# Attention scores on TensorE: even and odd heads in the lower and the upper 64 rows of the array, each with a PSUM bank of its own

## The chip, the cores and the metric

The kernel runs on one core of a Trainium2 chip. The metric is the device time of one execution in microseconds (us), as the median of several runs. The profile is one further execution, recorded by the hardware profiler; its span is the time from the first to the last recorded instruction of the core. TensorE stands in it as two engines: PE is the matmul itself and PEld the load of the stationary operand (LDWEIGHTS), which overlaps the matmul before it. The others are VectorE (DVE), ScalarE (ACT), GpSimd (POOL) and SyncE (SP), which issues the DMAs.

## The reference

Pooled attention over 4 batches, 8 heads, 576 tokens and a head size of 64, followed by two feed-forward layers over the 2304 tokens. All numbers are float32.

```
k_p = k.reshape(B, H, Sp, pool, D).mean(axis=3)          # pool = 8, Sp = 72
v_p = v.reshape(B, H, Sp, pool, D).mean(axis=3)
scores = scale * np.matmul(q, k_p.transpose(0, 1, 3, 2))
scores = scores - np.max(scores, axis=-1, keepdims=True)
attn = np.exp(scores)
attn = attn / (np.sum(attn, axis=-1, keepdims=True) + 1e-09)
x = np.matmul(attn, v_p)                                  # then to (2304 tokens, 512)
xn = x / sqrt(mean(x * x) + 1e-06) * rms_g
x = (silu(xn @ w_gate) * (xn @ w_val)) @ w_out            # 512 -> 1536 -> 512
h = x @ w_in;  y = silu(h) @ w_out                        # 512 -> 2048 -> 512
```

## The kernel before

The first tenth of the time is the attention; the rest are the two feed-forward layers, whose matmuls (line 2010 and the lines behind it) keep TensorE busy to the end. The change touches the attention alone.

The 2304 tokens are cut into 18 tiles of 128. A batch has 576 tokens, four and a half tiles, so tiles 4 and 13 hold tokens of two batches: `parts(n)` gives two parts of 64 tokens for them and one part of 128 for each other tile. The list `order`, written out at the start of the kernel, sets what each engine does; all engines walk through the same list. In step s it has: the scores of tile s, the transposes of tile s-1's probabilities (`prT`), the transposes of the queries of tile s+1 (`q`), the transposes of the normalized output of an earlier tile (`x`), for three tiles the transposes of a new batch's keys (`keys`), and the product with the values of tile s-1 (`pv`). So on TensorE one round is: scores (line 1909), `prT` (line 1921), `q` (line 1896), `x` (line 1953), `pv` (line 1940), and then the scores of the next tile.

The other engines work between these. ScalarE copies the transposed queries from PSUM to `qT` (line 1411) and the pooled keys to `kT` (line 1394), makes the exponentials in place in `pr` (line 1086) and copies their transpose to `prT` (line 1420). VectorE takes the maximum of the scores for each head (line 1487, into `mx`), subtracts it (line 1492, into `pr`), and divides the product with the values by the sums (lines 1507 to 1514). Semaphores order all this; `s_sc` counts the score tiles made, `s_shift` the tiles subtracted.

The scores of one part are four matmuls, one for each pair of heads c. The stationary operand is `qT[:, c, tokens]`: partitions 0 to 63 hold the 64 elements of the even head, 64 to 127 those of the odd head. The moving operand is a block of `kT` of 128 partitions and 144 columns, block-diagonal: the even head's 72 keys stand in the lower 64 partitions and columns 0 to 71, the odd head's in the upper 64 partitions and columns 72 to 143, and the other two quarters are zero. VectorE clears both `kT` buffers once at the start (line 1809) and the copies fill only the two quarters. The scores of heads 0 to 3 lie in PSUM bank 2 and those of heads 4 to 7 in bank 3. One float32 matmul of the code stands in the trace as two pairs of LDWEIGHTS and MATMUL, so the scores of a tile are 8 pairs, those of tiles 4 and 13 are 16.

In the trace, a TensorE instruction carries its rows and columns of the array: 128\*128 uses all of it, 128\*64 only 64 columns, as the matmuls for the 64-token parts of tiles 4 and 13 do, in the scores and in the product with the values.

Of the kernel before, what the change touches and what calls it, by code (L numbers as in the profile page):

```python
# [13 lines left out]
P = 128  # L14
# [6 lines left out]
def ffn_kernel(nc, q, k, v, w_gate, w_val, w_out, rms_g, w2_in, w2_out, out):  # L21
    B, H, S, D = q.shape
    DM = H * D
    KC = DM // P
    T = B * S
    SP = S // POOL
# [21 lines left out]
    def parts(n):  # L48
        at, found = n * P, []
        while at < (n + 1) * P:  # L50
            b = at // S
            end = min((b + 1) * S, (n + 1) * P)
            found.append((b, at - n * P, end - at))
            at = end
        return found

    order = [("q", 0)]
    for s in range(NT + 2):
# [228 lines left out]
    with ctx:  # L287
# [6 lines left out]
        def sem(name):  # L294
            return ctx.enter_context(nc.semaphore(name))
# [77 lines left out]
            vb.append(at(spot, f"vb{i}", [P, RC, HS, E]))  # L373
            spot += 4 * RC * HS * E
        for i in range(2):
            kT.append(at(spot, f"kT{i}", [P, R]))
            spot += 4 * R
        assert spot <= ring_at[2] + SLOT
        spot = c_at + RAW
        ident = at(spot, "ident", [P, P])  # L380
# [97 lines left out]
        o_ps = ps[:, 6:8, 0:HB * E].rearrange("p b (h e) -> p b h e", e=E)  # L478

        s_const, s_mask, s_ident = sem("const_made"), sem("mask_made"), sem("ident_made")  # L480
        s_pad0, s_pad, s_clear = sem("k0_pad_cleared"), sem("pad_cleared"), sem("kT_pr_cleared")
        s_q = [sem(f"q_loaded{i}") for i in range(2)]
        s_k = [sem(f"k_loaded{i}") for i in range(2)]
        s_v = [sem(f"v_loaded{i}") for i in range(2)]
# [40 lines left out]
        def _(sp):  # L525
# [31 lines left out]
            def load_raw(i):  # L557
                kind, x = made[i]
                if raw_before[i] is not None:
                    sp.wait_ge(s_wlo, raw_before[i] + 1)  # L560
                elif raw_of(i) == 2:
                    sp.wait_ge(s_sc, NT)
                elif made[i] == ("r", U2 + 1):

                    sp.wait_ge(s_flo, PART * 4)
                elif kind == "c" and CHOME[x] == 0:
                    sp.wait_ge(s_out, 16)
                elif kind == "c":
                    sp.wait_ge(s_down, down0[ND])
                    sp.wait_ge(s_ost[0], o_store[o_maker[GROUPS[1] + GROUPS[2] - 1]])  # L570
                    sp.wait_ge(s_ost[1], o_store[o_maker[GROUPS[1] + GROUPS[2] - 2]])
                elif raw_of(i) >= 7:
                    sp.wait_ge(s_prod, NF * (last_unit[0] + 1))
                elif raw_of(i) > 3:
                    sp.wait_ge(s_ksum, 3)
                    sp.wait_ge(s_vsum, 3)
                if made[i] in (("r", U2 + 2), ("o", N2)):
                    sp.wait_ge(s_wh, 2 * (NF - 1))
                if made[i] == ("c", 6):
                    sp.wait_ge(s_wh, 4 * NF)  # L580
                if kind == "b":

                    sp.dma_start(raw[raw_of(i)][:, :].rearrange("p (k n) -> p k n", k=2),
                                 w_out.rearrange("(k j p) n -> p j k n", p=P, k=2)[:, x, :, :])\
                      .then_inc(s_raw[raw_of(i)], 16)
                elif kind == "c":
                    sp.dma_start(raw[raw_of(i)][:, :].rearrange("p (k n) -> p k n", k=2),
                                 w2_out.rearrange("(k j p) n -> p j k n", p=P, k=2)[:, x, :, :])\
                      .then_inc(s_raw[raw_of(i)], 16)
                elif kind == "r":  # L590
                    ph, letter, g, _ = units[x]
                    sp.dma_start(raw[raw_of(i)][:, :].rearrange("p (c n) -> p c n", c=KC),
                                 up_v[letter][:, :, g * FF:(g + 1) * FF]).then_inc(s_raw[raw_of(i)], 16)
                else:
                    g = downs[x][1]
                    sp.dma_start(raw[raw_of(i)][:, :].rearrange("p (c n) -> p c n", c=2),
                                 down_v[ffn_of[x]][:, 2 * g:2 * g + 2, :]).then_inc(s_raw[raw_of(i)], 16)
# [485 lines left out]
        def _(act):  # L1083
# [302 lines left out]
            def keys(b):  # L1386

                act.wait_ge(s_kTm, b + 1)
                act.wait_ge(s_clear, 3)
                if b >= 2:  # L1390
                    act.wait_ge(s_sc, first_tile[b - 1] + 1)
                for e in range(2 if b else 1):
                    half = slice(e * D, (e + 1) * D)
                    last = act.activation(
                        kT[b % 2][half, :].rearrange("p (c e j) -> p c e j", e=2, j=SP)[:, :, e, :],
                        flat[half, 0:R].rearrange("p (c e j) -> p c e j", e=2, j=SP)[:, :, e, :], ACT.Copy)
                last.then_inc(s_kTc, 1)

# [7 lines left out]
            for what, n in order:  # L1406
                if what == "q":
                    act.wait_ge(s_qTm, n + 1)
                    if n >= 1:
                        act.wait_ge(s_sc, n)  # L1410
                    act.activation(qT[:, :, :], q_ps, ACT.Copy).then_inc(s_qTc, 1)
                    if n in first_tile:
                        keys(first_tile.index(n))
                    if n >= 1:
                        exp(n - 1)
                elif what == "prT":
                    act.wait_ge(s_pTm, n + 1)
                    if n >= 1:
                        act.wait_ge(s_o, n)
                    act.activation(prT[:, :, :], prT_ps, ACT.Copy).then_inc(s_pTc, 1)  # L1420
                    if n == NT - 2:
                        exp(NT - 1)
                    if n == NT - 1:
                        keep_first(0)
                elif what == "pv":
                    if n >= 2:
                        norm(n - 2)
                    if n >= 1:
                        squares(n - 1)
                    if n in (8, 9, 13):  # L1430
                        weight_high(0, ((8, 9, 13).index(n),))
                    if n in (15, 16, 17):
                        weight_high(made_at["r", 1], (n - 15,))
                elif what == "x" and 7 <= n < 7 + NF:
                    token_high(0, XORDER[n - 7])
                elif what == "unit":
                    act_unit(n)
# [25 lines left out]
        def _(dve):  # L1463
# [17 lines left out]

            def shift(n):
                scores = sc_ps.rearrange("p b (h j) -> p b h j", j=SP)
                dve.wait_ge(s_sc, n + 1)
                if n >= 1:
                    dve.wait_ge(s_shift, n)
                dve.tensor_reduce(mx[:, :].rearrange("p (b h) -> p b h", b=2), scores, AX.X, ALU.max)\
                   .then_inc(s_max, 1)
                dve.wait_ge(s_max, n + 1)
                if n >= 2:  # L1490
                    dve.wait_ge(s_pTm, n - 1)
                dve.tensor_tensor(pr[:, n % 2, 0:R].rearrange("p (b h j) -> p b h j", b=2, j=SP), scores,
                                  mx[:, :].rearrange("p (b h) -> p b h", b=2).unsqueeze(3)
                                  .broadcast_to([P, 2, HB, SP]), ALU.subtract).then_inc(s_shift, 1)

# [309 lines left out]
                    ending_low(ENDINGS.index(ph), 0, ((0, 1), (2, 3))[g - EPART - 1])  # L1805

            dve.memset(KV[0][0][LAST:P, RC - 1, :], 0.0).then_inc(s_pad0, 1)
            for i in range(2):
                dve.memset(kT[i][:, :], 0.0).then_inc(s_clear, 1)
            dve.memset(pr[:, :, R:RC * P], 0.0).then_inc(s_clear, 1)  # L1810
            for i in range(2):
                dve.wait_ge(s_kpart[i], 16)
# [2 lines left out]
            sum_rows(0, *KPARTS[2]).then_inc(s_kpartsum, 1)  # L1815

            dve.wait_ge(s_kTm, 1)
            dve.wait_ge(s_clear, 3)
            dve.tensor_copy(kT[0][D:2 * D, :].rearrange("p (c e j) -> p c e j", e=2, j=SP)[:, :, 1, :],
                            flat[D:2 * D, 0:R].rearrange("p (c e j) -> p c e j", e=2, j=SP)[:, :, 1, :])\  # L1820
               .then_inc(s_khalf, 1)
            for what, n in order:
# [53 lines left out]
        def _(pe):  # L1876
# [23 lines left out]
            def scores(n):  # L1900
                pe.wait_ge(s_qTc, n + 1)
                pe.wait_ge(s_kTc, parts(n)[-1][0] + 1)
                if n == 0:
                    pe.wait_ge(s_khalf, 1)
                else:
                    pe.wait_ge(s_shift, n)
                for b, r0, m in parts(n):
                    for c in range(KC):
                        last = pe.matmul(sc_ps[r0:r0 + m, c // 2, (c % 2) * 2 * SP:(c % 2 + 1) * 2 * SP],  # L1909
                                         qT[:, c, r0:r0 + m], kT[b % 2][:, c * 2 * SP:(c + 1) * 2 * SP],  # L1910
                                         start=True, stop=True)
                last.then_inc(s_sc, 1)

            def transpose_p(n):
                pe.wait_ge(s_exp, n + 1)
                pe.wait_ge(s_clear, 3)
                if n >= 1:
                    pe.wait_ge(s_pTc, n)
                pe.wait_ge(s_kTc, sum(1 for b in range(B) if first_tile[b] <= n + 1))
# [285 lines left out]
```

## Time and profile before

| | |
|---|---|
| time, median of 3 runs | 861.84 us (861.83 to 861.92) |
| the profiled execution's own time | 861.54 us |
| its span | 859.8 us |
| instructions in it | 13900 |
| PE busy | 850.9 us (99%) |
| PEld busy | 830.6 us (97%) |
| DVE busy | 551.4 us (64%) |
| ACT busy | 359.9 us (42%) |
| POOL busy | 422.4 us (49%) |
| data moved by DMA | 235.78 MB |

Busy time is the time in which at least one instruction of the engine is under way, from its start to its end; for PE that includes the time in which a result still runs through the array, so that overlapping matmuls are not counted twice.

### The profile page before, as it was taken

What the parts mean: (1) busy time and instruction counts of PE and PEld (TensorE: products, weight loads), DVE (VectorE), ACT (ScalarE), POOL (GpSimd) and SP (SyncE); (2) the same over time, 40 slices, a digit from 0 to 9 for tenths busy, and PEclk for the clock granted to TensorE, in tenths of its full rate; (3) what the DMA queues carried; (4) which work ended last, traced back from release to release, by engine and by line L of the source; (5) the groups of instructions that cost most, each with busy time, mean ns of one, the idle gap of its engine ahead of it and who ended that gap; (6) DMA issues with size and microseconds to landing.
All of it is one profiled execution on the core that took longest, in us unless ns stands there. A gap on an engine that the chain in (4) does not pass through costs nothing.

```text
span 859.8 us, 13900 instructions
## 1 busy us (share of the span) xinstructions
PE 850.9 (99%) x5292; PEld 830.6 (97%) x5292; DVE 551.4 (64%) x835; ACT 359.9 (42%) x640; POOL 422.4 (49%) x415
## 2 busy tenths in 40 slices
PE   7999999999999999999999999999999999999998
PEld 6999999999999999999899899999999999999998
DVE  6789757876545579965554345569634698335873
ACT  3689745443221335555553221324333444134521
POOL 6898999883427480577773044380161700004400
PEclk9999999999999999999999999999999999999999
DMA  9971578778869987565779489997789747687763
GB/s 266 277 203 39 221 267 325 269 297 315 335 213 405 409 327 264 201 262 221 282 289 370 160 295 363 356 401 266 265 288 359 255 188 285 248 335 244 257 232 114
DMA packets 95201, 235.78 MB, mean 274 GB/s; under 512 B 23072, under 2 KB 69920, under 8 KB 83616
## 3 DMA queue, kind: packets, MB, share of 16 engines
q1 hardware_dynamic: 95136, 234.90, 75.4%
q8 instruction: 42, 0.69, 0.3%
q14 instruction: 23, 0.19, 0.1%
HBM read 164.10 MB, written 70.78 MB: 273 GB/s over the span
## 4 chain that ended last, share of the span: by engine, by line
PE 97%; DVE 1%; DMA 1%; issue 0%; ACT 0%; SPq 0%; DVEq 0%
PE ps L2010 17%; PE ps L2012 17%; PE ps L2011 17%; PE ps L2148 5%; PE ps L2147 5%; PE ps L2146 5%; PE ps L1940 4%; PE ps L2106 3%; PE ps L2107 3%; PE ps L2108 3%; PE ps L2077 3%; PE ps L2078 3%; PE ps L2076 3%; PE ps L1909 2%; PE ps L2052 2%; PE ps L2053 2%
## 5 line engine op out<-in xcount | busy, mean ns | idle before, releaser
L2010 PE MATMUL ps<-xh,wr 128*128 128x384 f32 x840 | 283.2, 337 | 0.3
L2012 PE MATMUL ps<-xh,wr 128*128 128x384 f32 x840 | 281.4, 335 | 0.0
L2011 PE MATMUL ps<-xl,wr 128*128 128x384 f32 x840 | 281.2, 335 | 0.0
L2010 PEld LDWEIGHTS ps<-xh,wr 128*128 128x128 f32 x840 | 157.7, 188 | 4.4 <-DVE qt L1579 1.5
L2011 PEld LDWEIGHTS ps<-xl,wr 128*128 128x128 f32 x840 | 157.9, 188 | 0.3
L2012 PEld LDWEIGHTS ps<-xh,wr 128*128 128x128 f32 x840 | 157.7, 188 | 0.0
L2148 PE MATMUL ps<-ew,efl 128*128 128x256 f32 x336 | 95.2, 283 | 0.0
L2147 PE MATMUL ps<-ew,efh 128*128 128x256 f32 x336 | 95.2, 283 | 0.0
L2146 PE MATMUL ps<-ew,efh 128*128 128x256 f32 x336 | 95.2, 283 | 0.0
L1598 DVE TENSOR_TENSOR qt<-ps,qt 128x384 f32<-128x384 f32 x84 | 46.3, 556 | 49.8 <-PE ps L2012 49.7
L959 POOL TENSOR_TENSOR eh<-eh 128x768 f32<-128x768 f32 x8 | 17.2, 2168 | 122.5 <-DVE efl L1675 122.5
L2148 PEld LDWEIGHTS ps<-ew,efl 128*128 128x128 f32 x336 | 64.6, 192 | 0.0
L2146 PEld LDWEIGHTS ps<-ew,efh 128*128 128x128 f32 x336 | 64.6, 192 | 0.0
L2147 PEld LDWEIGHTS ps<-ew,efh 128*128 128x128 f32 x336 | 64.6, 192 | 0.0
L1188 ACT ACTIVATE qt<-ps 128x384 f32<-128x384 f32 x42 | 20.6, 492 | 101.4 <-PE ps L2012 100.9
L1675 DVE TENSOR_TENSOR efl<-eh,efh 128x768 fp32r<-128x768 f32 x56 | 59.8, 1123 | 5.1 <-ACT efh L1288 5.1
L939 POOL TENSOR_TENSOR ebt<-raw_z 128x256 f32<-128x256 f32 x8 | 5.9, 737 | 112.7 <-PE ps L2108 39.9
L1288 ACT ACTIVATE efh<-eh 128x768 fp32r<-128x768 f32 x56 | 43.0, 834 | 41.3 <-PE ps L2148 41.3
L2106 PE MATMUL ps<-fh,fw 128*128 128x384 f32 x168 | 56.2, 334 | 0.0
L2107 PE MATMUL ps<-fl,fw 128*128 128x384 f32 x168 | 56.2, 334 | 0.0
L2108 PE MATMUL ps<-fh,fw 128*128 128x384 f32 x168 | 56.2, 334 | 0.0
L1587 DVE TENSOR_TENSOR qt<-ps,qt 128x384 f32<-128x384 f32 x42 | 23.4, 558 | 51.0 <-PE ps L2012 51.0
(198 smaller groups left out, 1769.0 us busy)
## 6 DMA issues: line engine op xcount, KB each, us to landing
wr<-ring_home SPq DMA_DIRECT2D x40, 1792.0 KB, 9.7
ring_home<-wr SPq DMA_DIRECT2D x20, 1792.0 KB, 8.1
ew<-ending_home SPq DMA_DIRECT2D x8, 2048.0 KB, 8.5
out_home<-wo SPq DMA_DIRECT2D x14, 1024.0 KB, 9.4
fw<-fold_home SPq DMA_DIRECT2D x8, 1536.0 KB, 7.8
ew<-out_home SPq DMA_DIRECT2D x24, 512.0 KB, 7.5
fw<-out_home SPq DMA_DIRECT2D x18, 512.0 KB, 6.6
ending_home<-eb SPq DMA_DIRECT2D x16, 512.0 KB, 10.7
```

The source lines that it names most:

```text
L1288: act.activation(efh[e][i % 2][:, 2 * j:2 * j + 2, :], ending_part(f, j), ACT.Copy).then_inc(s_ehi, 1)
L1598: dve.tensor_tensor(done if units[u][1] == "V" else qt[:, c, :], done, tiles(u)[:, c, :], ALU.add)\
L1675: dve.tensor_tensor(efl[e][i % 2][:, 2 * j:2 * j + 2, :], ending_part(f, j), efh[e][i % 2][:, 2 * j:2 * j + 2, :], ALU.subtract).then_inc( ...
L2010: pe.matmul(out_ps, w_hi, x_hi, start=first and c == 0, stop=False, skip_group_check=True)
L2011: pe.matmul(out_ps, w_hi, x_lo, start=False, stop=False, skip_group_check=True)
L2012: ins = pe.matmul(out_ps, w_lo, x_hi, start=False, stop=c == 1, skip_group_check=True)
L2106: pe.matmul(out_ps, w_hi, h_hi, start=first and c == 0, stop=False, skip_group_check=True)
L2107: pe.matmul(out_ps, w_hi, h_lo, start=False, stop=False, skip_group_check=True)
L2108: ins = pe.matmul(out_ps, w_lo, h_hi, start=False, stop=c == 2 * PART - 1, skip_group_check=True)
L2146: pe.matmul(out_ps, h_hi, w_hi, start=first and c == 0, stop=False, skip_group_check=True)
L2147: pe.matmul(out_ps, h_hi, w_lo, start=False, stop=False, skip_group_check=True)
L2148: ins = pe.matmul(out_ps, h_lo, w_hi, start=False, stop=c == 2 * EPART - 1, skip_group_check=True)
```

## The change

Each of the four score matmuls of a part becomes two, one for the even head (e = 0) and one for the odd head (e = 1). A matmul takes only the 64 partitions of its head, of `qT` and of `kT`, and makes 72 columns instead of 144. The even head's operands lie in partitions 0 to 63 and so in the one half of the array's rows, the odd head's in the other half. Even heads' scores go to PSUM bank 2 and odd heads' to bank 3.

`kT` keeps only the filled quarters: it is 4 × 72 columns wide in each half of the partitions instead of 8 × 72, its copies write 288 columns in a row, and the two clears of line 1809 go. The subtraction reads the scores bank by bank as before but writes `pr` in the order of the heads, with jumps of 72. `s_sc` now rises by two for each part (once for each bank), and `scored(n)` gives the count that stands for n tiles.

```diff
+    def scored(n):
+        return sum(2 * len(parts(i)) for i in range(n))
...
-            kT.append(at(spot, f"kT{i}", [P, R]))
-            spot += 4 * R
+            kT.append(at(spot, f"kT{i}", [P, HB * SP]))
+            spot += 4 * HB * SP
...
                 act.wait_ge(s_kTm, b + 1)
-                act.wait_ge(s_clear, 3)
...
                     last = act.activation(
-                        kT[b % 2][half, :].rearrange("p (c e j) -> p c e j", e=2, j=SP)[:, :, e, :],
+                        kT[b % 2][half, :].rearrange("p (c j) -> p c j", j=SP),
                         flat[half, 0:R].rearrange("p (c e j) -> p c e j", e=2, j=SP)[:, :, e, :], ACT.Copy)
...
-                dve.wait_ge(s_sc, n + 1)
+                dve.wait_ge(s_sc, scored(n + 1))
...
-                dve.tensor_tensor(pr[:, n % 2, 0:R].rearrange("p (b h j) -> p b h j", b=2, j=SP), scores,
+                dve.tensor_tensor(pr[:, n % 2, 0:R].rearrange("p (h b j) -> p b h j", b=2, j=SP), scores,
...
-            for i in range(2):
-                dve.memset(kT[i][:, :], 0.0).then_inc(s_clear, 1)
...
                 for b, r0, m in parts(n):
                     for c in range(KC):
-                        last = pe.matmul(sc_ps[r0:r0 + m, c // 2, (c % 2) * 2 * SP:(c % 2 + 1) * 2 * SP],
-                                         qT[:, c, r0:r0 + m], kT[b % 2][:, c * 2 * SP:(c + 1) * 2 * SP],
-                                         start=True, stop=True)
-                last.then_inc(s_sc, 1)
+                        for e in range(2):
+                            ins = pe.matmul(sc_ps[r0:r0 + m, e, c * SP:(c + 1) * SP], qT[e * D:(e + 1) * D, c, r0:r0 + m],
+                                            kT[b % 2][e * D:(e + 1) * D, c * SP:(c + 1) * SP], start=True, stop=True)
+                            if c == KC - 1:
+                                ins.then_inc(s_sc, 1)
```

Nothing changes its place in the order of an engine. On TensorE this is the place from the product with the values of tile 3 over the scores of tile 5 to the transposes behind them, in the kernel before (the form is output columns of a matmul of the code: partitions of the output x moving columns):

```order
L1940 MATMUL ps<-vb,prT 128x65
L1909 MATMUL ps<-kT,qT 128x144 [waits shifted,kT_copied,qT_copied]
L1909 MATMUL ps<-kT,qT 128x144 x3
L1921 MATMUL ps<-ident,pr 128x128 [waits prT_copied,kT_copied,kT_pr_cleared,exp_made]
```

The same place in the changed kernel, in which line 1909 has become 1911, 1921 has become 1923 and 1940 has become 1942:

```order
L1942 MATMUL ps<-vb,prT 128x65
L1911 MATMUL ps<-kT,qT 128x72 [waits shifted,kT_copied,qT_copied]
L1911 MATMUL ps<-kT,qT 128x72 x7
L1923 MATMUL ps<-ident,pr 128x128 [waits prT_copied,kT_copied,pr_cleared,exp_made]
```

And the scores of tile 4 in the changed kernel, the first of the two tiles that are cut into two parts (before, these were 8 matmuls `64x144`):

```order
L1911 MATMUL ps<-kT,qT 64x72 [waits shifted,kT_copied,qT_copied]
L1911 MATMUL ps<-kT,qT 64x72 x15
```

Four matmuls of 144 columns have become eight of 72, behind the same waits and between the same neighbours; for the two cut tiles, eight have become sixteen.

## Rows read from the trace of the kernel before

**Rows 1.** The page: busy time of the engines, granted clock in 40 slices, chain by engine

```profile
PE 850.9 (99%) x5292; PEld 830.6 (97%) x5292; DVE 551.4 (64%) x835; ACT 359.9 (42%) x640; POOL 422.4 (49%) x415
...
PEclk9999999999999999999999999999999999999999
...
PE 97%; DVE 1%; DMA 1%; issue 0%; ACT 0%; SPq 0%; DVEq 0%
```

**Rows 2.** The chain in order of time, one round: start us, us, what

```profile
56.13 1.69 PE ps L1940 x12
57.82 1.04 PE ps L1909 x8
```

**Rows 3.** The chain, around the matmuls that use 64 of the array's columns

```profile
25.09 1.50 PE ps L1940 x12
26.59 1.67 PE ps L1909 x16
28.27 0.70 PE ps L1921 x5
...
36.42 1.18 PE ps L1909 x8
37.60 0.55 PE ps L1921 x5
...
67.10 1.67 PE ps L1909 x16
...
76.93 1.18 PE ps L1909 x8
```

**Rows 4.** The timeline, single instructions: start us, us, engine, line, operation

```profile
57.49 0.19 PEld L1940 LDWEIGHTS ps<-vb,prT 128*128 128x128 f32 x1
57.60 0.19 PEld L1909 LDWEIGHTS ps<-kT,qT 128*128 128x128 f32 x1
...
26.32 0.27 PE L1940 MATMUL ps<-vb,prT 128*128 128x65 f32 x1
26.52 0.13 PEld L1909 LDWEIGHTS ps<-kT,qT 128*64 128x64 f32 x1
...
36.35 0.19 PEld L1909 LDWEIGHTS ps<-kT,qT 128*128 128x128 f32 x1
```

**Rows 5.** All instructions of line 1909: ns min/median/max, starts, forms

```profile
L1909 PE MATMUL ps<-kT,qT x160: 285/286/390, 10.3 to 86.1; 128*128 128x144 f32 x128, 128*64 128x144 f32 x32
```

**Rows 6.** The timeline of PEld: eight loads of a plain tile, eight of a cut one

```profile
53.45 1.04 PEld L1909 LDWEIGHTS ps<-kT,qT 128*128 128x128 f32 x8
...
26.94 0.56 PEld L1909 LDWEIGHTS ps<-kT,qT 128*64 128x64 f32 x8
```

**Rows 7.** The chain at the start of the kernel

```profile
10.27 1.23 PE ps L1909 x8
...
12.32 0.77 DVE pr L1492
...
15.74 0.30 issue
16.05 1.74 PE ps L1940 x12
```

**Rows 8.** The timeline of VectorE at the start of the kernel

```profile
1.63 1.15 DVE L1809 MEMSET kT<- 128x576 f32 x2 [0.18 <-issue]
...
3.44 1.05 DVE L1465 TENSOR_REDUCE kvp<-kv 128x64 f32<-128x512 f32 x1 [0.52 <-DMA kv<-in_k]
...
13.13 1.97 DVE L1465 TENSOR_REDUCE kvp<-kv 128x128 f32<-128x1024 f32 x1
```

**Rows 9.** VectorE and ScalarE in a round, then busy time of 50 to 80 us (PE, PEld, DVE, ACT, POOL)

```profile
55.68 0.76 DVE L1492 TENSOR_TENSOR pr<-ps,mx 128x576 f32<-128x576 f32 x1
...
56.47 0.69 ACT L1086 ACTIVATE pr<-pr 128x576 f32<-128x576 f32 x1
...
50.00:80.00 30.00, 29.56 (x245) 27.89 (x244) 29.31 (x46) 25.91 (x51) 27.10 (x32) 1.00 0.49 134
```

More of the change, by code:

```diff
@@ L480, in ffn_kernel @@
         s_const, s_mask, s_ident = sem("const_made"), sem("mask_made"), sem("ident_made")
-        s_pad0, s_pad, s_clear = sem("k0_pad_cleared"), sem("pad_cleared"), sem("kT_pr_cleared")
+        s_pad0, s_pad, s_clear = sem("k0_pad_cleared"), sem("pad_cleared"), sem("pr_cleared")
         s_q = [sem(f"q_loaded{i}") for i in range(2)]
@@ L561, in load_raw @@
                 elif raw_of(i) == 2:
-                    sp.wait_ge(s_sc, NT)
+                    sp.wait_ge(s_sc, scored(NT))
                 elif made[i] == ("r", U2 + 1):
@@ L1388, in keys @@
                 act.wait_ge(s_kTm, b + 1)
-                act.wait_ge(s_clear, 3)
                 if b >= 2:
-                    act.wait_ge(s_sc, first_tile[b - 1] + 1)
+                    act.wait_ge(s_sc, scored(first_tile[b - 1] + 1))
                 for e in range(2 if b else 1):
@@ L1409, in _ @@
                     if n >= 1:
-                        act.wait_ge(s_sc, n)
+                        act.wait_ge(s_sc, scored(n))
                     act.activation(qT[:, :, :], q_ps, ACT.Copy).then_inc(s_qTc, 1)
@@ L1817, in _ @@
             dve.wait_ge(s_kTm, 1)
-            dve.wait_ge(s_clear, 3)
-            dve.tensor_copy(kT[0][D:2 * D, :].rearrange("p (c e j) -> p c e j", e=2, j=SP)[:, :, 1, :],
+            dve.tensor_copy(kT[0][D:2 * D, :].rearrange("p (c j) -> p c j", j=SP),
                             flat[D:2 * D, 0:R].rearrange("p (c e j) -> p c e j", e=2, j=SP)[:, :, 1, :])\
@@ L1908, in scores @@
                     for c in range(KC):
-                        last = pe.matmul(sc_ps[r0:r0 + m, c // 2, (c % 2) * 2 * SP:(c % 2 + 1) * 2 * SP],
-                                         qT[:, c, r0:r0 + m], kT[b % 2][:, c * 2 * SP:(c + 1) * 2 * SP],
-                                         start=True, stop=True)
-                last.then_inc(s_sc, 1)
+                        for e in range(2):
[3 more added lines that the diff above has]
+                                ins.then_inc(s_sc, 1)
             def transpose_p(n):
                 pe.wait_ge(s_exp, n + 1)
-                pe.wait_ge(s_clear, 3)
+                pe.wait_ge(s_clear, 1)
                 if n >= 1:
```

## The prediction

> **What bounds the kernel now.** I read the page first: PE is busy for 850.9 of 859.8 us, the chain of work that ended last lies on PE for 97%, and the granted clock is full in every slice [rows 1]. So TensorE sets the end, and a nanosecond that it gains or loses in a stretch without waits is one of the whole. Next I read the chain in order of time through the attention. In a plain round the pieces of PE follow one another without a gap, and the scores are one of them: 1.04 us for 8 pairs of load and matmul [rows 2]. There are 18 such stages between 10 and 87 us. Then I looked for what the trace shows of the array in another shape, because the change puts every score matmul into a new one (64 rows). Rows for that exist: the cut tiles 4 and 13 use 64 of 128 columns, and the chain and the single instructions there tell what it costs to enter and leave a shape, and whether two parts of the array work at the same time [rows 3, 4, 6]. Last, the first two tiles, where PE waits for others [rows 7, 8], and the other engines [rows 9].
>
> **Price of a pair before.** Eight loads of the scores take 1.04 us from the first start to the last end; less the 0.19 of the last, seven steps of 0.12 [rows 4, 6]. A record of a matmul has 286 ns [rows 5], since it includes the way through the array; the step is what counts. The matmuls have 144 columns, so a column costs 0.122/144 = 0.85 ns and the eight take 0.98; the remaining 0.06 of the 1.04 is the end of the first load, which nothing covers [rows 2]. The load of 128 columns has a price of its own: two follow each other after 57.60 - 57.49 = 0.11 us, where the matmuls between them have only 65 columns [rows 4]. The whole stage of line 1940 agrees: its columns (four times 195, 130 and 65) would take 1560 × 0.85 ns = 1.33 us, the chain has 1.50 where it doesn't wait [rows 3], so four short matmuls take 0.10 each instead of 0.055. A matmul of 72 columns costs 0.061 and is thus bound by its load, whose 128 columns (tokens) are what they were.
>
> **Price of a pair after.** A tile has 16 pairs, in two streams of 8, one for each half of the rows. No row shows a matmul on 64 rows. Bounds: if only the columns counted and the halves worked side by side, 8 × 0.061 = 0.49 us; if all 16 loads stood in one line, 15 × 0.11 + 0.06 = 1.71. The nearest rows are those of tile 4, whose two parts use different halves of the columns: eight loads take 0.56 us there [rows 6], (0.56 - 0.13)/7 = 0.06 a step [rows 4, 6] for matmuls of 144 columns that cost 0.12 each in a single stream, so the two halves do work side by side. I take the same for halves of the rows, with each stream bound by its loads: 7 × 0.11 + 0.06 = 0.83 instead of 0.98, **-0.15 us** for each stage.
>
> **Price of the change of shape.** The trace shows it in three kinds. Going from the full array to 64 columns, the first load of the scores starts 0.20 us after the last matmul before it (26.32 to 26.52), while in a plain round it starts 0.11 after the load before it, under running matmuls [rows 4]: the array is emptied first, and the load is then uncovered. Going from 64 columns to the full array with a load of 128 columns, the score stage takes 1.18 instead of 1.04, twice [rows 2, 3]: **+0.14**. Going from 64 columns back to the transposes of line 1921, their stage takes 0.70 instead of 0.55 [rows 3]: **+0.15**. After the change every score stage stands between stages on the full array (line 1940 before, line 1921 behind) and pays both. The Trainium skill says so too ("TensorEngine Tiling (Array Packing)", Key Properties): changing the tiling mode, not only the tile, drains TensorE. By that rule, the trace agrees for columns; for rows no run here shows it. Without it the sum below would be the rival with -3.8 us.
>
> **The sum.** Twelve plain stages (tiles 2, 3, 5, 7 to 12, 14, 16, 17): -0.15 + 0.14 + 0.15 = +0.14 each, **+1.7**. Tiles 6 and 15, at 36.42 and 76.93, enter from 64 columns already, since the product of the cut tile stands before them [rows 3]: -0.15 + 0.15 = **0**. Tiles 4 and 13 pay both changes already, and their loads have 64 columns, about 0.06 us, as their matmuls: 1.67 is 0.15 to enter and 1.52 for 16 pairs, against 1.96 in one line, so the second part began 0.54 us after the first, 4.4 of its 8 pairs [rows 3]. After, each part runs as two streams of 8 × 0.061 = 0.49, and with the same lead of 4.4 pairs (0.27) the stage takes 0.76 instead of 1.52: -0.76 each (bounds: no overlap of the parts -0.54, full overlap -1.03), **-1.5**. Tile 0: PE is idle before it, so entering is free, and leaving falls into the wait for VectorE; the 0.15 goes on through its subtraction [rows 7]: **-0.15**, or nothing if the value sum at 13.13 waits for its load [rows 8]. Tile 1 gains 0.15 and loses it on leaving, and behind it are 0.30 of waiting for VectorE anyway [rows 7]: 0. Sum: +1.7 - 1.5 - 0.15 = +0.05 us. The profiled execution took 861.54 us, so 861.6; it lies 0.3 under the median of the runs, so in their terms **861.9 us**.
>
> **What costs nothing.** The two clears of `kT` took 1.15 us, but VectorE then waits 0.52 for the keys' DMA, which ends when it ends [rows 8]. The copies to `kT` have as many elements. The subtraction writes with jumps of 72; it took 0.76 [rows 9], the maximum, which reads in runs of 72, takes about the same. It ends at 56.44, its tile's exponentials at 57.16, and PE asks for them with the scores at 57.60 and with line 1921 after them: 1.1 us and, one score stage later, about 1.4 us of cover. If it took over 1 us longer, PE would wait in every round. VectorE is busy for 29.31 of 30 us between 50 and 80 [rows 9], so PE could gain little more there than that cover; in the forecast PE gains nothing there before tile 13.
>
> **The rivals.**
> (a) The halves' loads stand in one line: one port feeds the stationary operand. For it: no row shows two row halves at once. Against: the loads of two column halves overlap [rows 6]. Body 1.71 instead of 0.98, +0.73: twelve stages × (0.73 + 0.29) = +12.2, tiles 6 and 15 +1.8, the cut tiles 32 × 0.061 = 1.95 instead of 1.52, +0.9, the first two some +1.3: +16.2, **878.1 us**, slower. It decides from a body of 0.95 us on: 14 stages × 0.12 make 1.7 us, what a measurement can tell.
> (b) Loads overlap but the moving columns don't: 16 × 0.061 = 0.98, no gain against the two changes of shape. 12 × 0.29 + 2 × 0.15 + 0.9 = +4.7, **866.6 us**, slower.
> (c) Going to 64 rows and back empties nothing. Then 14 × -0.15 - 1.5 - 0.15 = -3.75, **858.1 us**. Against it is every change of shape that the trace has.
> (d) A load of 64 rows takes half, and columns bind: body 0.49. 12 × (0.29 - 0.49) + 2 × (0.15 - 0.49) - 1.5 - 0.5 = -5.1, **856.8 us**. For it: 64 columns make a load shorter (0.13 against 0.19 [rows 4]); but those are columns, and here they stay 128. The Trainium skill's table ("TensorEngine Tiling (Array Packing)", Theoretical Speedup) promises up to 2× where a small dimension is at most 64, which would be this case; its page on TensorE ("TensorE: Matmul & The Clock Gate", LDWEIGHTS) says that a load's time goes by columns, not rows, which speaks for my 0.83.
>
> **How the numbers follow.** A measurement of this kernel tells about 0.2% (1.7 us) from no change. Forecast 0.47, with its own range 860.5 to 863.5 (body ±0.06 in 14 stages, cut tiles ±0.25 each); (a) 0.17; (b) 0.10; (c) 0.15; (d) 0.07; 0.04 for what I don't see. The range 856.5 to 868.0 leaves out (a) and a little. Faster is (c), (d) and 0.03 of the forecast: 0.25. Slower is (a), (b), 0.04 of the forecast and half of the rest: 0.33. Same: 0.42.
>
> **What would show it.** In the chain after, line 1911 takes about 1.03 us in a plain round (0.20 to enter, 0.83 body) and line 1923 0.70; 1.91 would be (a), 0.89 with 0.55 behind it (c). Loads of line 1911 come in twos, 0.11 from two to two. The cut tiles' stage takes about 0.9. The stages after 100 us keep their length. I am wrong if row halves don't behave as column halves do, which no row can tell me.

## The result: 2.1 us longer

The changed kernel takes 863.95 us (median of 21 executions, 861.87 to 865.13), the kernel before 861.85 in as many (860.95 to 863.21). The ratio is 1.0018, with a 95% interval of 1.0012 to 1.0024. That is a real loss of 2.1 us, at the edge of the 0.2% that the prediction called no change, and forty times the +0.05 of its sum. The profiled execution took 864.21 us (span 862.5), so it stands 0.3 above its median; the one of before, 861.54, stood 0.3 under its own. One execution of one experiment below (`e2_before_fill`) took 926.14 us with a mean granted clock of 0.852; it is left out.

The page after, the lines that answer to [rows 1]:

```profile
PE 854.0 (99%) x5452; PEld 832.4 (97%) x5452; DVE 550.3 (64%) x833; ACT 359.8 (42%) x640; POOL 421.2 (49%) x415
...
PEclk8999999999999999999999999999999999999999
...
PE 95%; DVE 3%; issue 1%; DMA 1%; ACT 0%; SPq 0%; DVEq 0%
```

Three things differ. There are 160 more matmuls, as written. The first digit of the granted clock is 8 where it was 9. And VectorE holds 3% of the chain, where it had 1%. The prediction had neither the second nor the third.

The chain after, in order of time: the start, the first cut tile (4), one plain round, and the end of the attention (start us, us, what):

```profile
10.10 1.14 PE ps L1911 x16
...
12.05 0.77 DVE pr L1495
12.82 0.14 issue
12.96 1.97 PE ps L1911 x16
14.93 1.26 PE ps L1923 x5
...
17.04 3.08 PE ps L1942 x12
20.12 1.05 PE ps L1911 x16
...
29.25 0.96 PE ps L1911 x27
30.21 0.69 PE ps L1923 x5
...
36.09 2.44 PE ps L1942 x22
38.53 1.05 PE ps L1911 x16
39.58 0.69 PE ps L1923 x5
...
56.28 1.04 PE ps L1911 x16
57.32 0.70 PE ps L1923 x5
...
86.47 0.68 DVE xacc L1503
87.15 1.99 DVE xl L1559
...
95.46 1.58 PE ps L1942 x12
```

Lines have moved: 1911, 1923 and 1942 are the 1909, 1921 and 1940 of before. The plain round is as forecast: scores 1.04 as in [rows 2], line 1923 0.70 instead of 0.55 [rows 3]. The cut tile's scores take 0.96 where they took 1.67 [rows 3]. But between 12.96 and 20.12 every stage takes nearly twice its usual time: 1.97 against 1.05, 1.26 against 0.70, 3.08 against about 1.7. The busy time by stretch says why. Columns: stretch, its length, busy us and instructions of PE, PEld, DVE, ACT, POOL, granted clock, DMA share, GB/s. First after, then before:

```profile
9.00:13.00 4.00, 2.20 (x26) 1.63 (x23) 1.98 (x3) 1.59 (x4) 3.15 (x5) 1.00 1.20 255
13.00:19.60 6.60, 6.60 (x35) 6.13 (x36) 4.11 (x4) 2.47 (x4) 2.82 (x5) 0.50 1.16 279
```

```profile
13.00:19.60 6.60, 5.75 (x46) 5.54 (x46) 5.94 (x9) 2.76 (x5) 3.59 (x6) 1.00 1.14 305
```

The granted clock is 0.50 for 6.6 us, the lower of its two levels (1.2 GHz), and TensorE gets through 35 matmuls in it instead of 46, though those of the scores are now half as wide. Before it fell, TensorE had stood still: the scores of tile 0 and the transposes of line 1896 were done at 11.8, and the scores of tile 1 waited for VectorE until 12.96 (the chain's 0.77 of `pr`). But the kernel before has that wait too, and a slightly longer one. The timelines of PE, before and after, with the idle time in brackets, and the busy time of 9 to 13 us before, to set beside the first row above:

```profile
13.23 1.22 PE L1909 MATMUL ps<-kT,qT 128*128 128x144 f32 x8 [1.30 <-DVE pr L1492]
...
12.96 1.97 PE L1911 MATMUL ps<-kT,qT 64*128 64x72 f32 x16 [1.16 <-DVE pr L1495]
```

```profile
9.00:13.00 4.00, 2.28 (x16) 1.64 (x14) 1.90 (x3) 1.50 (x3) 3.29 (x5) 1.00 1.21 276
```

TensorE waited for 1.30 us before and for 1.16 after, and in the four microseconds it was busy for 2.28 and 2.20. So neither the wait nor the busy time tells the two kernels apart; what differs up to there is above all how the scores of tile 0 are made.

The other place is 87.15. Subtracting `xl` on VectorE took 1.99 us of the chain. The same operation on the same tile, with GpSimd's subtraction beside it, in the timelines of before (first fence) and after:

```profile
84.49 0.95 DVE L1556 TENSOR_TENSOR xl<-xt,xh 128x768 fp32r<-128x768 f32 x1
84.51 2.06 POOL L900 TENSOR_TENSOR wr<-wt,wr 128x512 fp32r<-128x512 f32 x1
```

```profile
87.05 1.27 POOL L904 TENSOR_TENSOR wr<-wt,wr 128x512 fp32r<-128x512 f32 x1
87.07 2.07 DVE L1559 TENSOR_TENSOR xl<-xt,xh 128x768 fp32r<-128x768 f32 x1
```

Before, VectorE began 0.02 us ahead of GpSimd, took 0.95, and GpSimd took 2.06. After, GpSimd began 0.02 ahead, took 1.27, and VectorE took 2.07. They don't share the time; the later one waits. Its time is nearly the rest of the first one's and its own in a row: 1.25 + 0.95 = 2.20 us for the 2.07 of VectorE, and 0.93 + 1.27 = 2.20 for the 2.06 of GpSimd. The Trainium skill has this rule ("SBUF — State Buffer", SBUF: two separate sides): VectorE and GpSimd share one pair of ports, "an exclusive lock, not a bandwidth split", and the one that starts first holds it for its whole instruction. By that rule, both traces agree on who waits, though a lead of 0.02 us decides it; the waiting one ends 0.13 to 0.14 us earlier than a full wait would make it.

**Where 2.67 us between the profiled executions lie.** I read the start of each tile's scores in both timelines. The first scores start 0.17 earlier after (10.10 against 10.27; over all traces here they start between 9.87 and 10.60, whatever the kernel). From tile 0 to tile 2, where the clock is low, 9.95 us instead of 7.35: +2.60. (Two traces of this kind of kernel with the full clock, `e1_fill` and `e12_after_tiny` below, take +0.26 and +0.22 there, so about 2.4 of it are the clock's.) From tile 2 to tile 17, 67.94 instead of 67.58: +0.36. From tile 17 to the last product with the values (before it started at 92.00, after at 95.46), 7.47 instead of 6.80: +0.67, behind the late `xl`. Together 3.46. The rest of the kernel gives 0.79 back, where TensorE waits for others anyway: the distance between the traces is 3.55 us at 127 us, 3.43 at 248, 3.13 at 515 and 2.73 at 776. It shrinks at three places of the kernel before (at 179, 482 and 564 us), by about 0.3 us at each.

### The profile page after: what moved, and what is told of

It is laid out like the page before. It is cut to its first block, busy times and chain, and to the rows that moved or that the text cites. A ratio compares the mean times of both kernels' runs of the same rounds, so it can differ in the third digit from the quotient of the medians.

```text
span 862.5 us, 14215 instructions
## 1 busy us (share of the span) xinstructions
PE 854.0 (99%) x5452; PEld 832.4 (97%) x5452; DVE 550.3 (64%) x833; ACT 359.8 (42%) x640; POOL 421.2 (49%) x415
## 4 chain that ended last, share of the span: by engine, by line
PE 95%; DVE 3%; issue 1%; DMA 1%; ACT 0%; SPq 0%; DVEq 0%
PE ps L2012 17%; PE ps L2014 17%; PE ps L2013 17%; PE ps L2150 5%; PE ps L2149 5%; PE ps L2148 5%; PE ps L2110 3%; PE ps L2109 3%; PE ps L2108 3%; PE ps L1942 3%; PE ps L2079 3%; PE ps L2080 3%; PE ps L2078 3%; PE ps L2055 2%; PE ps L2054 2%; PE ps L2053 2%
```

## Experiments

Each is the changed kernel or the one before with the edit shown. The median of before that stands beside each was taken on the same chip at the same time.

### The cut tiles alone, and the plain tiles alone

`e3_cut_only` scores only tiles 4 and 13 on half rows; the others keep the block-diagonal `kT` and the full array. `e4_plain_only` is the reverse.

```diff
+    def halves(n):
+        return len(parts(n)) == 2
...
+                if not halves(n):
+                    for b, r0, m in parts(n):
+                        for c in range(KC):
+                            last = pe.matmul(sc_ps[r0:r0 + m, c // 2, (c % 2) * 2 * SP:(c % 2 + 1) * 2 * SP],
+                                             qT[:, c, r0:r0 + m], kT[b % 2][:, c * 2 * SP:(c + 1) * 2 * SP],
```

> Only the two cut tiles (4 and 13) make their scores on half the rows; the other 16 are as before, with the block-diagonal keys. By the sum of the prediction this keeps the -0.76 us of each cut tile and none of the changes of shape of the others. Theory: the cut stage takes 0.96 us instead of 1.67, tile 4 gives 0.7 us whole, tile 13 gives 0.2 to 0.7 as VectorE is nearly full there, and the start is as before, so the clock too: 860.4 to 861.0 us, faster than before by 0.1 to 0.17%. Rival (VectorE binds everything behind 50 us): what tile 4 gains is lost there, and the time is 861.6 to 861.9 us, no change. If the writes of the scores in another order cost VectorE something, it shows here in the two tiles only.

> The other part alone: the 16 plain tiles on half the rows, the two cut ones as before. Theory (clock and sum): +0.14 us in each of 12 tiles, nothing in 6 and 15 and at the start, so +1.5 us by the sum with the clock kept, and another 2 us in executions that lose the clock: 863.3 us without the loss, 865.3 with it. Rival (VectorE): the stages of PE are longer but covered by nothing, so the same +1.5 us without any fall of the clock and then no two kinds of executions.

Measured: cut tiles alone 862.28 us (before 861.49; ratio 1.0009, 1.0000 to 1.0018), plain tiles alone 863.97 (1.0026, 1.0016 to 1.0037). The plain tiles lose, as the sum says of them, but this median doesn't size the sum: six of its seven executions have a mean granted clock of 0.996 or 0.998. From tile 2 to tile 17, behind the low clock, its trace takes 68.88 us instead of 67.58, +1.3 where the sum has +1.5 for the eleven stages between (this trace has no collision of `xl`). In it the low clock lasts only half as long as in the changed kernel's, about 3.4 us, and tile 0 to tile 2 takes 0.97 us more than before instead of 2.60:

```profile
13.20:16.50 3.30, 3.30 (x23) 2.89 (x20) 3.17 (x4) 0.87 (x2) 1.43 (x3) 0.50 1.09 331
16.60:20.00 3.40, 3.40 (x35) 3.26 (x35) 2.21 (x5) 1.28 (x2) 1.88 (x2) 1.00 1.21 257
```

The cut tiles should have gained some 0.8 us and did not: a miss. The trace of `e3_cut_only` shows two places where the gain goes. The chain around tile 4 runs through GpSimd, and shortly ahead of tile 17 the collision is there again (chain, then timeline):

```profile
28.08 1.55 POOL kv L849
...
29.72 0.87 POOL kvp L859
...
33.51 2.51 PE ps L1956 x22
...
92.34 1.57 PE ps L1956 x12
```

```profile
83.92 1.28 POOL L906 TENSOR_TENSOR wr<-wt,wr 128x512 fp32r<-128x512 f32 x1
83.94 2.08 DVE L1562 TENSOR_TENSOR xl<-xt,xh 128x768 fp32r<-128x768 f32 x1
```

TensorE saves 0.71 us in the step from tile 4 to tile 5 (4.13 instead of 4.84), but the sums of keys and values that GpSimd makes until 30.6 pace what follows, and the next step takes 5.44 instead of 4.99: 0.45 of it goes back. At tile 17 the kernel is 0.40 us ahead (74.53 us behind its first scores instead of 74.93), and from there to the last product it takes 7.73 instead of 6.80. The profiled execution is a fast one, though: 861.54 us, as the profiled one of before, and 0.74 under its median.

### The collision: one tiny GpSimd operation

`e8_cut_tiny` is `e3_cut_only`, `e12_after_tiny` the changed kernel, each with a clear of one column ahead of GpSimd's last subtraction, so that it starts a little later.

```diff
                     pool.tensor_tensor(w[:, 1, 3:5, :, :], t[:, 0:2, :, :], w[:, 0, 3:5, :, :], ALU.subtract)
+                    if i == 0:
+                        pool.memset(tiny[:, :], 0.0)
```

> e3_cut_only with one more instruction: a clear of one column (about 0.1 us) on GpSimd between its two last subtractions on the first weights. In the trace of e3_cut_only TensorE is 0.59 us ahead of before at the scores of tile 17, and 0.4 us behind after the attention; in between one VectorE subtraction (xl) takes 2.08 us instead of 0.95, which began 0.02 us after a subtraction of GpSimd (83.94 against 83.92), while in before it began 0.02 us ahead of it (84.49 against 84.51) and GpSimd's took 2.06 instead of 1.28. Theory (order of two engines on one port): with GpSimd 0.1 us later, VectorE goes first, its subtraction takes 0.95, and the 1.1 us come back: 860.3 to 860.9 us, about 1 us under e3_cut_only. Rival (end of the attention paced by ScalarE or by the weights): the subtraction gets shorter but the time stays at 862 us. Rival (the gain of the cut tiles is lost in VectorE anyway): 861.5 us.

> The changed kernel with GpSimd's small clear alone, without the eight transposes. Theory: the clock falls as in the changed kernel, in most executions (granted mean 0.996 to 0.998), and the subtraction is short: 862.7 to 863.3 us, 1 us under the changed kernel and 1 to 1.5 over e10_both. Rival (the fall of the clock is what makes VectorE late, and the two costs are one): 861.5 to 862.3 us, as e10_both.

The timeline of `e8_cut_tiny`:

```profile
84.42 0.95 DVE L1565 TENSOR_TENSOR xl<-xt,xh 128x768 fp32r<-128x768 f32 x1
...
84.38 0.11 POOL L908 MEMSET tiny<- 128x1 f32 x1
84.43 2.08 POOL L909 TENSOR_TENSOR wr<-wt,wr 128x512 fp32r<-128x512 f32 x1
```

VectorE is 0.01 us ahead again and takes 0.95; the 2.08 is GpSimd's. From tile 17 to the last product the kernel takes 6.78 us, where `e3_cut_only` took 7.73. At the end of the kernel the two traces show nothing of that (861.60 and 861.54 us), so here the medians of 11 have to tell. The median is 861.02 (before 861.51; 0.9995, 0.9986 to 1.0004), against 862.28 without the clear and an expected 860.3 to 860.9. `e12_after_tiny` takes 6.85 us over that piece, where the changed kernel took 7.47. Its median is 863.27 (before 861.55; 1.0015, 1.0005 to 1.0024), and it falls into two groups: four executions with a mean granted clock of 1.0 took 861.18, 861.27, 861.30 and 862.47, seven with 0.996 took 863.19 to 864.12. So it parts the two costs by itself. With the collision gone, what is left is the clock: some 2.2 us between the groups. The changed kernel's 21 executions fall apart in the same way: the six at 1.0 have a median of 862.3, the five at 0.998 of 862.75, the ten at 0.996 of 864.4. At an equal clock and against their own kernels before, the clear is thus worth 0.6 us (0.996) and 0.7 (1.0), with few executions in each group.

The reverse, a tiny clear on VectorE in the kernel before, ahead of its `xl`, missed its place:

```diff
+                    if n == 13:
+                        dve.memset(tiny[:, :], 0.0)
```

> The kernel before with a clear of one column (under 0.1 us) on VectorE ahead of the subtraction xl that began 0.02 us before GpSimd's subtraction. Theory (who comes first has the port): VectorE now comes second and its subtraction takes 2.08 instead of 0.95 us; TensorE has about 0.4 us of cover at the end of the attention there, so 0.6 to 1.1 us are added: 862.1 to 862.6 us. Rival (the order of the two makes no difference to the end): 861.5 us, as before.

Measured 861.36 us (before 861.55; 0.9998, 0.9989 to 1.0007). In the trace the clear runs at 90.07, one tile too late, and `xl` at 86.04 still takes 0.95. The expected 862.1 to 862.6 is missed because the edit didn't do what it was for. It is inconclusive, and that the kernel before would lose the same by the same push wasn't shown.

### The clock: fill the idle stretch

`e1_fill` adds eight transposes, which write a bank that nothing reads then, behind the transposes of tile 1's queries; `e2_before_fill` does so in the kernel before.

```diff
                 if what == "q":
                     transpose_q(n)
+                    if n in (1,):
+                        for _ in range(8):
+                            pe.transpose(ps[:, 7, 0:P], ident[:, :], ident[:, :])
```

> The changed kernel with eight more transposes of the identity into the still unused bank 7, behind the query transposes of tile 1, where TensorE has nothing to do from 11.7 to 13.0 us. Theory (clock): the time beyond the forecast comes from the granted clock, which fell to half from 13.0 to 19.6 us behind that idle stretch. With the stretch filled it stays at 1.00, scores of tile 1 take 1.2 instead of 1.97 us, and the time is 861.5 to 862.3 us, 2 us under the changed kernel. Rival (VectorE): the extra time comes from VectorE, which the chain after shows from 66.7 to 93 us; then the filling changes nothing and the time stays at 863.5 to 864.5 us. Rival (work on half the rows counts less): the clock falls anyway, a little later, and the time stays over 863 us.

> The kernel before with the same eight transposes. Its profile shows the clock at 1.00 throughout, with the same idle stretch of 1.5 us. Theory (clock): the filling is worth nothing in the executions like the profiled one, so 861.5 to 862.0 us, within 0.1% of before; if some executions of before lose the clock too (its runs reach from 860.95 to 863.21), those go and the spread gets narrower. Rival (VectorE): no change at all, spread included.

Measured: 862.46 us (before 861.49; 1.0009, 1.0000 to 1.0018), a little over the expected 861.5 to 862.3, and 861.38 for the kernel before with them (ten executions; 0.9999, 0.9990 to 1.0008). The windows and the timeline of `e1_fill`:

```profile
13.00:19.60 6.60, 5.76 (x62) 5.30 (x60) 5.94 (x9) 2.44 (x5) 3.50 (x6) 1.00 1.15 301
```

```profile
11.49 1.04 PE L2162 MATMUL ps<-ident 128*128 128x128 f32 x8
12.81 0.89 PE L1911 MATMUL ps<-kT,qT 64*128 64x72 f32 x12 [0.28 <-DVE pr L1495]
```

The idle time ahead of tile 1's scores is 0.28 us instead of 1.2, the granted clock stays at 1.00 in all 11 executions, and TensorE does 62 matmuls in the stretch where it did 35. The transposes cost nothing, since they lie in the wait. The same collision as in the changed kernel remains in its trace: 7.48 us from tile 17 to the last product.

`e6_from_2` asks for the cause in another way: tiles 0 and 1 keep the full rows (`return n >= 2` in the function above), all others are on half rows.

> Tiles 0 and 1 as before (full rows), tiles 2 to 17 on half the rows. The stretch with idle time before the clock fell (11.7 to 13.0 us) is then as in before. Theory (clock): what TensorE does in tile 0 and 1 decides; the clock stays at 1.00 in all or nearly all executions, as in before, and the time is that of e1_fill, 861.7 to 862.8 us. Rival (half rows count as less work wherever they are): the clock falls in later stages, 20 to 60 us, and the time stays at 863.5 to 864.5 us.

862.82 us (before 861.51; 1.0017, 1.0008 to 1.0026), clock 1.0 in all 11 executions, with nothing in the wait. The low clock is thus a product of the two first tiles. All runs agree on that. Where tiles 0 and 1 are on half rows and nothing fills the wait, 32 of 43 executions have a mean clock below 1.0 (15 of 21 of the changed kernel, 7 of 11, 6 of 7 and 4 of 4 in `e12_after_tiny`, `e4_plain_only` and `e5_outer`). With the filling it is 0 of 22, and with full rows in these tiles 0 of 55 (`e6_from_2` and the four runs that change only the cut tiles). `e4_plain_only` still makes the two clears of `kT` and has its full width, so these are not the cause. The ratio stays high, since this trace has the collision too (`xl` 2.07 us; 7.47 to the last product).

`e10_both` is the changed kernel with the transposes and the clear:

> The changed kernel with the eight transposes (e1_fill) and GpSimd's small clear (e8_cut_tiny) together. Theory: the clock stays at 1.00 and VectorE's subtraction takes 0.95, so what is left is the sum of the prediction, +0.05 us on TensorE, +0.3 in the profile of e1_fill at tile 17: 861.4 to 861.9 us, no difference from before. Rival (the change has another cost of its own that these two don't hold): over 862.3 us.

Its trace has the full clock from the start to the last product, and no collision (VectorE, then GpSimd):

```profile
85.89 0.95 DVE L1562 TENSOR_TENSOR xl<-xt,xh 128x768 fp32r<-128x768 f32 x1
...
85.90 2.07 POOL L907 TENSOR_TENSOR wr<-wt,wr 128x512 fp32r<-128x512 f32 x1
```

861.78 us (before 861.55; 1.0002, 0.9993 to 1.0011). Against their own kernels before, the four kernels of this square stand at +2.10 us (changed), +1.72 (clear), +0.97 (transposes) and +0.23 (both). So the transposes give back 1.1 us alone and 1.5 beside the clear, the clear 0.4 alone and 0.7 beside the transposes. Each of these medians is uncertain by some 0.5 to 0.8 us, so the square alone doesn't size the clear. The traces do so up to the last product (0.62 us, 7.47 against 6.85), and at the end of the kernel the groups of equal clock above (0.6 and 0.7).

### The order of issue, and the two parts of a cut tile

`e5_outer` issues all even heads, then all odd ones:

```diff
-                    for c in range(KC):
-                        for e in range(2):
+                    for e in range(2):
+                        for c in range(KC):
```

> The changed kernel with all four even heads first and then the four odd ones, instead of turn about. Theory (each half of the array takes its own stream, TensorE looks about 4 pairs ahead, as in the cut tiles of before): the odd stream begins about 4.4 pairs of 0.11 us after the even one, so the body is 0.83 + 0.48 = 1.3 us instead of 0.83, +0.5 us for each of 16 stages, about +7 us, 871 us. Rival (the halves work side by side only if TensorE gets them turn about): body 1.71, +0.88 a stage, 877 us. Rival (it looks far enough ahead): no change, 864 us.

872.14 us (four executions; before 861.51; 1.0125, 1.0111 to 1.0138). Its chain:

```profile
55.86 1.55 PE ps L1911 x16
57.40 0.70 PE ps L1923 x5
```

The stage takes 1.55 instead of 1.04, +0.51. With pairs at 0.11, the second stream starts some 4.5 pairs later. The two halves of the rows do work side by side, but only as far as the order of TensorE's instructions lets the second one start. From tile 2 to tile 17 that makes 75.19 us instead of 67.94, 7.2 of the 8.2 between the medians (872.14 - 863.95).

`e7_inter` puts that to use in the cut tiles. It is `e3_cut_only` with the tile's two parts taken in turn, in the scores and in the product with the values:

```diff
-                for b, r0, m in parts(n):
-                    for c in range(KC):
+                for c in range(KC):
+                    for b, r0, m in parts(n):
...
-                for b, r0, m in parts(n):
-                    for bank in range(2):
...
+                        for i, (c, lo, hi) in enumerate(jobs):
+                            for b, r0, m in parts(n):
```

> e3_cut_only with the two parts of a cut tile taken turn about instead of one behind the other, in the scores (four streams of 8 pairs) and in the product with the values (two streams of 12). Theory (streams side by side): the cut score stage falls from 0.96 to about 0.7 us, the product stage from 2.44 to about 1.7 us, together 1.0 us for each cut tile on TensorE; tile 4's part of it goes through to 60 us, tile 13's is covered by VectorE, which is full from 66 us on. So 860.5 to 861.5 us if the end of the attention is bound by VectorE. Rival (streams of one kind already overlap as far as they can): stages as in e3_cut_only, 862.3 us.

```profile
24.66 3.02 POOL kv L845 x2
...
27.76 1.56 POOL kv L849
...
33.18 1.56 PE ps L1956 x24
34.75 1.18 PE ps L1916 x8
```

861.57 us (before 861.51; 1.0003, 0.9994 to 1.0012), at the upper edge of the expected 860.5 to 861.5. The product of a cut tile takes 1.56 us instead of 2.51 in `e3_cut_only`, and the scores' matmuls start within 0.51 us instead of 0.81. But the product starts at 33.18 because GpSimd's sums and what follows them end there, and the collision is there as well (`xl` 2.07, 7.72 to the last product). `e11_inter_tiny` adds GpSimd's clear to it:

> e7_inter, whose trace has the longer subtraction too (2.07 us, begun 0.01 us behind GpSimd's), with GpSimd's small clear. TensorE is 1.0 us ahead of before at tile 17 there. Theory: the 1.1 us come back and the end of the attention follows VectorE: 860.4 to 860.8 us, 0.8 to 1.1 us under e7_inter and under before. Rival: 861.5, as e7_inter, if ScalarE or GpSimd bound the end.

861.19 us (before 861.55; 0.9996, 0.9987 to 1.0005), against an expected 860.4 to 860.8: partly a miss. The collision is gone (`xl` 0.95, 6.78 to the last product), and TensorE reaches tile 17 at 74.42 us behind its first scores, 0.5 ahead of before. The expectation had counted 1.0 us from the start of the span in the trace of `e7_inter`; 0.40 of that was only that its first scores came earlier (9.87 against 10.27 us), which changes from one execution to the next. In the trace the lead reaches the end (860.87 us against 861.54 in the profiled execution of before), but the medians are only 0.36 apart. The two best versions, this one and `e8_cut_tiny`, are at 0.9996 and 0.9995, which no interval here tells from the kernel before.

## Why the prediction was right and wrong

**A plain stage (+0.14): right.** Entering costs what it did for columns: the chain shows 1.04 where 0.83 + 0.20 = 1.03 was expected, and leaving shows 0.70. In a run with the clock kept (`e12_after_tiny`) a plain round takes +0.15 to +0.17 more than before, where nobody waits. The prediction had weighed a rule of the Trainium skill there ("TensorEngine Tiling (Array Packing)", Key Properties): a change of mode drains TensorE. By that rule, the trace agrees for halves of the rows as well, with the 1.04 and the 0.70.

**Two streams (body 0.83): right.** The timeline of PEld after:

```profile
56.21 0.19 PEld L1911 LDWEIGHTS ps<-kT,qT 64*128 64x128 f32 x2
...
56.21 0.97 PEld L1911 LDWEIGHTS ps<-kT,qT 64*128 64x128 f32 x16
```

Two loads lie side by side within one 0.19, and sixteen end after 0.97: 0.19 + 7 × 0.11. The sixteen matmuls start within 0.84 us, the eight of before within 0.91. That refutes rival (a), which wanted 1.71, rival (b), and rival (d), since a load of 64 rows is not shorter (median 188 ns). Rival (c) fell with the 0.70.

**Cut tiles (-0.76 each): the stage right, the worth of tile 4 only in part of the runs.** 1.67 became 0.96, close to the 0.91. At tile 13 the steps from tile 12 to 14 take 0.67 us less than before when the clock is kept, against -0.62 by the sum (-0.76 and +0.14). At tile 4 the step gives 0.61. The next step keeps that in the traces of the changed kernel, `e1_fill` and `e6_from_2` (+0.07 to +0.08), and takes 0.41 back in `e12_after_tiny` (5.40 instead of 4.99). There the load of the values landed at 24.92, GpSimd's sums began at 25.22, 0.3 later than in `e1_fill`, and they pace TensorE. Its chain runs from that load over the sums to the product:

```profile
17.82 7.10 DMA kv<-in_v
...
25.22 3.05 POOL kv L844 x2
...
33.78 2.52 PE ps L1945 x22
```

So whether the gain of tile 4 comes through hangs on a transfer. The low clock has no part in it, since `e1_fill` kept its clock. The prediction had read no row of GpSimd between 24 and 33 us, and took that stretch for one without waits.

**Tile 0 (-0.15) and tile 1 (0): the step that failed.** The prediction costed the two first tiles with the durations of a full clock and booked a shorter stage as a gain. Instead the clock fell behind tile 0 in most executions, and in the profiled one tile 0 to tile 2 took 2.60 us more. Of the 21 executions, 15 have a mean granted clock below 1.0; the other six have 1.0, and four of those took 861.87 to 862.55 (the other two 864.47 and 864.55, for which I have no cause). Of 89 executions of before whose clock is on record, 88 have 1.0; the one at 0.998 took 863.31, the longest of them all. So the kernel before can lose the clock as well, but hardly ever does. The fall is shown to depend on how tiles 0 and 1 are made (`e6_from_2`), and filling the wait ahead of tile 1 prevents it (`e1_fill`). The wait by itself is not the cause, as before has it too. Whether the shorter work or the half rows let the clock fall was not separated. With the clock kept, the -0.15 didn't come either: the value sum, which began at 13.13 in [rows 8], waited for its load (0.28 us in `e12_after_tiny`, 0.32 in `e1_fill`), which is the condition that the prediction had named for "nothing".

**The subtraction of `xl`: not in the sum.** The prediction spoke of VectorE's cover of 1.1 to 1.4 us, and asked only whether its own operations would grow. What grew, by 1.1 us, was an operation that the change doesn't touch, because the meeting of two engines shifted by 0.04 us. Up to the last product it costs 0.62 us in the changed kernel (7.47 against 6.85), and 0.95 with the cut tiles alone (7.73 against 6.78). That it happens in every execution of the changed kernel is not shown; only the profiled ones can be looked at.

**The whole.** With both disturbances taken out, the change is worth +0.2 us (`e10_both`, 1.0002, 0.9993 to 1.0011), which agrees with the +0.05 that was forecast. That agreement is partly luck, because the path through the attention did not come out as summed. In `e12_after_tiny`, with the full clock and a short `xl`, TensorE takes 0.94 us more than before from tile 0 to tile 17 (75.87 against 74.93), where the sum has about -0.1 for that stretch. Of the difference, 0.37 lies in tiles 0 and 1, 0.41 is what tile 4 gave back, and the rest is spread over the other stages. Behind the attention its trace is 0.61 us behind that of before, with its first scores 0.38 earlier, and at the end 0.25 ahead: the three waits at 179, 482 and 564 us take back nearly 0.9. The prediction said that "a nanosecond that it gains or loses in a stretch without waits is one of the whole", but it had looked for no wait behind 100 us. The stages after 100 us kept their length, as expected; only the waits between them shrank. The time fell inside the range 856.5 to 868.0, and outside the forecast's own 860.5 to 863.5. The range was that wide for the rivals (a) to (d), none of which was at work, so that it held the time is luck too. The 0.04 for "what I don't see" was too little for two such effects, each about as large as the largest term of the sum.

## What to carry to other kernels

A stage of 1 us on half rows between stages on the full array pays about 0.3 us for the two changes of shape, so the packing must save more than that in it. Where such stages can be grouped, one pair of changes would serve several; that was not tried here. Taking only those that change shape anyway lost nothing, but no interval shows that it gained. Issue the halves in turn. Before booking a gain, look for waits further on that may take it back, and at what else is timed by the moved engine: an idle stretch of TensorE near the start, and pairs of VectorE and GpSimd operations that start within some hundredths of a microsecond of each other in a stretch where VectorE is full.

## What was unexpected of the hardware

- The granted clock fell to 0.50 for 6.6 us in one profiled execution and for 3.4 us in another, behind a wait of about 1.2 us of TensorE in the first 13 us of the kernel, in most executions and not in all. The kernel before has a wait of 1.30 us at the same place in its trace, and 88 of its 89 executions on record have a mean clock of 1.0. Eight transposes in the wait (1.04 us, no cost) kept it at 1.00 in all 11.
- Which of two subtractions, one on VectorE and one on GpSimd, starts 0.01 to 0.02 us earlier decides whether VectorE's takes 0.95 or 2.07 us. GpSimd's takes 2.06 or 1.27 in return.
- Streams on different halves of the rows run side by side when they are issued in turn (sixteen loads in 0.97 us), and 0.51 us later when issued one behind the other.
